# Recurrent attention in 64-token chunks with soft and dense MLP behind it: a round's products and transposes in another order

## The reference

```python
for t in range(S):                                   # the part that the change concerns
    cur = einsum('bhd,bhe->bhde', u * k[t], v[t])
    y[t] = einsum('bhd,bhde->bhe', r[t], state + cur)
    state = w[t][..., None] * state + einsum('bhd,bhe->bhde', k[t], v[t])
x = y as (3072, 384)
x = soft mixture of 8 experts (x, phi, w1, w2)       # softmax over tokens in, over slots out
out = relu(x @ w_in) ** 2 @ w_out                    # 3072 x 384
```

## Time and profile before

| | us |
|---|---|
| median of 3 runs | 546.54 (543.76 to 552.49) |
| the profiled execution | 547.0 |
| its span | 545.2 |
| attention rounds | from about 5 to 236 |
| mean granted clock of TensorE | 0.974 of full |

### The profile page before, as it was taken

One profiled execution on the slowest core, in us unless ns is written; L12 is line 12 of the kernel. 1 busy time (PEld: TensorE's weight loads), 2 busy tenths in 40 slices (PEclk: granted clock), 3 DMA queues, 4 the chain that ended last, 5 costly groups with the idle time before them and its releaser, 6 DMA issues.

```text
span 545.2 us, 18788 instructions
## 1 busy us (share of the span) xinstructions
PE 483.3 (89%) x7850; PEld 423.2 (78%) x7850; DVE 334.7 (61%) x583; ACT 332.6 (61%) x689; POOL 13.7 (3%) x21
## 2 busy tenths in 40 slices
PE   5868979798979798778798789999999999999996
PEld 3657768677867676777334289999999999999996
DVE  8687878786878788644441276555555555555552
ACT  4777686867777778353213276656565656565653
POOL 9000000000000000000000000000000000000000
PEclk9998999998999999789899979999999999999999
DMA  8775484846362624862999430101010101010101
GB/s 168 131 166 118 95 199 79 203 84 112 63 111 57 110 47 121 274 190 60 315 400 373 173 115 1 45 1 44 1 44 2 43 0 44 0 44 0 44 1 43
DMA packets 129388, 56.24 MB, mean 103 GB/s; under 512 B 103328, under 2 KB 128928, under 8 KB 128928
## 3 DMA queue, kind: packets, MB, share of 16 engines
q1 hardware_dynamic: 126112, 54.53, 38.1%
q10 hardware_dynamic: 3200, 0.59, 0.6%
HBM read 50.38 MB, written 4.72 MB: 101 GB/s over the span
## 4 chain that ended last, share of the span: by engine, by line
PE 74%; ACT 13%; issue 7%; DVE 3%; SPq 1%; ACTq 1%; DMA 0%; DVEq 0%
PE bank L730 12%; PE bank L732 12%; PE bank L731 12%; PE lbank L474 5%; ACT wide L825 5%; PE ybank L508 5%; PE bank L720 4%; PE ybank L524 4%; PE tbank L425 4%; PE lbank L491 3%; PE bank L669 2%; PE bank L646 2%; PE tbank L438 2%; ACT wl L766 2%; PE ybank L455 1%
## 5 line engine op out<-in xcount | busy, mean ns | idle before, releaser
L730 PE MATMUL bank<-wo_high,h_high 128*128 128x384 f32 x384 | 129.4, 337 | 1.6 <-DVE h_low L1228 1.4
L731 PE MATMUL bank<-wo_low,h_high 128*128 128x384 f32 x384 | 128.9, 336 | 0.0
L732 PE MATMUL bank<-wo_high,h_low 128*128 128x384 f32 x384 | 128.9, 336 | 0.0
L974 ACT ACTIVATE h_relu<-bank 128x384 f32<-128x384 f32 x128 | 62.9, 491 | 74.2 <-PE bank L720 73.7
L1226 DVE CAST h_high<-h_sq 128x384 fp32r<-128x384 f32 x128 | 46.0, 359 | 96.4 <-PE bank L732 87.7
L1062 DVE TENSOR_TENSOR rk<-rk,wl 112x768 f32<-112x768 f32 x80 | 76.2, 952 | 37.2 <-PE lbank L474 24.6
L730 PEld LDWEIGHTS bank<-wo_high,h_high 128*128 128x128 f32 x384 | 72.6, 189 | 3.0 <-issue 2.5
L1228 DVE TENSOR_TENSOR h_low<-h_sq,h_high 128x384 fp32r<-128x384 f32 x128 | 71.5, 558 | 4.4
L731 PEld LDWEIGHTS bank<-wo_low,h_high 128*128 128x128 f32 x384 | 72.5, 189 | 0.0
L732 PEld LDWEIGHTS bank<-wo_high,h_low 128*128 128x128 f32 x384 | 72.5, 189 | 0.0
L978 ACT ACTIVATE h_sq<-h_relu 128x384 f32<-128x384 f32 x128 | 67.4, 527 | 4.1
(11 more groups left out here) (123 smaller groups left out, 517.5 us busy)
## 6 DMA issues: line engine op xcount, KB each, us to landing
w_sb<-in_moe_w_dram SPq DMA_DIRECT2D x32, 384.0 KB, 5.3
w_hi<-in_moe_w_dram SPq DMA_DIRECT2D x16, 384.0 KB, 9.0
v_tok<-in_v_dram SPq DMA_DIRECT2D x32, 144.0 KB, 3.0
w_lo<-in_moe_w_dram SPq DMA_DIRECT2D x1, 4608.0 KB, 16.4
out_dram<-o_sb SPq DMA_DIRECT2D x8, 576.0 KB, 3.0
nat<-in_r_dram SPq DMA_DIRECT2D x62, 72.0 KB, 2.5
nat<-in_k_dram SPq DMA_DIRECT2D x62, 72.0 KB, 2.7
nat<-in_w_dram SPq DMA_DIRECT2D x60, 72.0 KB, 2.5
```

Source lines behind the costliest of these rows:

```text
L730: nc.tensor.matmul(acc, hi, wo_high[:, fb, :], start=(fb == 0), stop=False)
L731: nc.tensor.matmul(acc, hi, wo_low[:, fb, :], start=False, stop=False)
L732: last = nc.tensor.matmul(acc, lo, wo_high[:, fb, :], start=False, stop=(fb == NF - 1))
L974: nc.scalar.activation(h_relu[fb % 2][:], h_bank[fb % 2][:, 0:GT * P], ACT.Relu).then_inc(relu_done, 1)
```

## The change

The program text of PE, ACT and DVE is put in another order; no operation is added, removed or resized.

- PE: the near product of pair 0 moves from behind level 3 of pair 0 up to before level 2 of pair 1, its far product from behind level 3 of pair 1 to behind level 3 of pair 0, the near product of pair 1 from behind level 4 of pair 1 to before level 4 of pair 0, its far product from behind level 5 of pair 0 to behind level 4 of pair 1. The units slip down: unit 3 behind level 2 of pair 1, 5 behind level 3 of pair 0, 6 behind level 3 of pair 1, 7 behind level 4 of pair 0, 8 behind level 4 of pair 1, 9 and 10 behind level 5 of pair 0, and 11 behind level 5 of pair 1, the last thing of a round.
- ACT: its copies follow in the same order. Unit 11's copies now stand behind both pairs' level-5 copies, between those of pair 1 and the widening of pair 1.
- DVE: update 0 of pair 1 moves from the end of a round to the beginning of the next, behind merge 0 of pair 0.

```diff
@@ tensor, in the loop over rd
                 level(rd, 0, 2)
-                next_inputs(rd, 2, 2)
+                next_inputs(rd, 2, 1)
+                if late:
+                    y_near(rd - 1, 0)
                 level(rd, 1, 2)
-                next_inputs(rd, 4, 2)
+                next_inputs(rd, 3, 2)
                 level(rd, 0, 3)
                 if late:
-                    y_near(rd - 1, 0)
+                    y_far(rd - 1, 0)
+                next_inputs(rd, 5, 1)
+                level(rd, 1, 3)
                 next_inputs(rd, 6, 1)
-                level(rd, 1, 3)
                 if late:
-                    y_far(rd - 1, 0)
+                    y_near(rd - 1, 1)
+                level(rd, 0, 4)
                 next_inputs(rd, 7, 1)
-                level(rd, 0, 4)
-                next_inputs(rd, 8, 2)
                 level(rd, 1, 4)
                 if late:
-                    y_near(rd - 1, 1)
-                next_inputs(rd, 10, 1)
+                    y_far(rd - 1, 1)
+                next_inputs(rd, 8, 1)
                 level(rd, 0, 5)
-                if late:
-                    y_far(rd - 1, 1)
+                next_inputs(rd, 9, 2)
+                level(rd, 1, 5)
                 next_inputs(rd, 11, 1)
-                level(rd, 1, 5)
@@ scalar, the end of the loop over rd
-                top_level_out(rd, 0)
                 if late:
                     y_to_x(rd - 1, 1)
-                if ahead:
-                    inputs_out(rd + 1, 11, 1)
+                next_out(8, 1)
+                top_level_out(rd, 0)
+                next_out(9, 2)
                 if ahead:
                     widen(rd + 1, 0, 1)
                 top_level_out(rd, 1)
+                next_out(11, 1)
                 if ahead:
                     widen(rd + 1, 1, 1)
@@ vector
             for rd in range(ROUNDS):
-                for s in range(2):
-                    merge(rd, s, 0)
+                merge(rd, 0, 0)
+                if rd > 0:
+                    update(rd, 1, 0)
+                merge(rd, 1, 0)
...
                 for s in range(2):
                     update(rd, s, 5)
-                    if rd < ROUNDS - 1:
+                    if s == 0 and rd < ROUNDS - 1:
                         update(rd + 1, s, 0)
```

More of the change, by code:

```diff
@@ L863, in _, with next_out @@
                 late = rd > 0
+                def next_out(first, count):
+                    if ahead:
+                        inputs_out(rd + 1, first, count)
                 if late:
                     k_out(rd - 1, 0)
-                if late:
                     k_out(rd - 1, 1)
-                if late:
                     kv_out(rd - 1, 0)
-                if ahead:
-                    inputs_out(rd + 1, 0, 1)
+                next_out(0, 1)
                 widen(rd, 0, 2)
@@ L874, in _ @@
                     kv_out(rd - 1, 1)
-                if ahead:
-                    inputs_out(rd + 1, 1, 1)
+                next_out(1, 1)
                 widen(rd, 1, 2)
-                if ahead:
-                    inputs_out(rd + 1, 2, 2)
+                next_out(2, 1)
                 widen(rd, 0, 3)
-                if ahead:
-                    inputs_out(rd + 1, 4, 2)
+                next_out(3, 2)
                 widen(rd, 1, 3)
-                if ahead:
-                    inputs_out(rd + 1, 6, 1)
                 if late:
                     y_to_x(rd - 1, 0)
-                if ahead:
-                    inputs_out(rd + 1, 7, 1)
+                next_out(5, 2)
                 for s in range(2):
                     spread_w(rd, s)
[L892 to L895, removed]
-                top_level_out(rd, 0)
+                next_out(7, 1)
                 if late:
                     y_to_x(rd - 1, 1)
-                if ahead:
-                    inputs_out(rd + 1, 11, 1)
+                next_out(8, 1)
+                top_level_out(rd, 0)
+                next_out(9, 2)
                 if ahead:
```

## The result

| | before | after |
|---|---|---|
| median, us | 546.56 | 566.03 (564.51 to 566.93) |
| ratio | | 1.0353 (95% interval 1.0311 to 1.0394) |
| span of the profiled execution | 545.2 | 563.9 |
| mean granted clock | 0.974 | 0.940 |

A forecast was written before the change was run, and what follows sets the result against it. It took each attention round's end, a chain of small steps on three engines, as the bound, not PE work. Terms 8.5 + 0 - 0.6 = +7.9 on 547.0 gave 554.9, stated as 555.0 us; range 546 to 563.

The forecast's parts named there:

- The tail as a chain: Level-4 merge of pair 1 to next level 1 of pair 0: 8.45 us each, +8.5 over seven rounds' ends.
- The middle: Level 1 to level 4 of pair 0: +1.06 work against 1.07 waits, about 14 us unchanged; term 0, bounds ±0.5 a round.
- clock as before: Case of longer round ends at unchanged granted clock: 554.9 us by the sum, 551 to 559, chance 0.48.
- The clock: Rival, left out of the sum: clock falls at every round's end, +3 to +8.5 us, middle 560.6 us; chance 0.28.
- The last round: No units there; the near product covers a 0.96 us wait between levels 2: -0.6 us, ends -2.3 and +0.5.
- The issue pauses fall into idle time: TensorE pauses (0.95 and 1.38) that lengthened old round ends fall into idle time in new ones; already within the +8.5.
- gains win: Rival: rounds' ends are not the bound, removed waits are won, about 1.4 x 6 = 8 us: 539 us; chance 0.08.

The follow-up runs named there:

- the run with the pauses filled: Changed kernel with 14 and 7 identity transposes, read by nobody, added in the two TensorE pauses of each round's end: 552.70 us, 1.0141 of the kernel before.
- with the next one filled: Changed kernel with only the second pause of each round's end filled, by 7 identity transposes ahead of pair 1's k transposes: 555.60 us, 1.0165 of the kernel before.
- unit 11 alone: Kernel before with only unit 11 put behind level 5 of pair 1, its copies and update as in the change: 564.49 us, 1.0342.
- unit 11 back: Changed kernel with only unit 11, its copies and update put back to their old places: 552.57 us, 1.0127 of the kernel before.

## Why the prediction was wrong

- **The tail as a chain: right.** The sum was 8.45; with the clock held up it is 8.40 to 8.46 in seven tails, and in round 3 of the changed kernel each step up to the widening of pair 1 came within 0.02 us. What TensorE does inside it was read less well: it was busy 5.09 of the 7.48 us of the old tail, not "some 3 to 4".
- **The middle: nearly right at full clock.** I took 14.0, from one round, and had +1.06 of work against 1.07 of waits. The six rounds of before have 14.38 on the mean; with the clock held up it is 13.76, so the term was -0.6 a round, just past my bound of -0.5, and not 0.
- **The sum for "clock as before": near, with some luck.** 554.9 forecast, 552.70 measured where the pauses are filled. The profiled execution of that run, 550.66, has a span 3.7 longer than before and not 7.9, mostly for the middle term.
- **The clock: the step that failed.** "In the sum I leave it out and make a case of it", on the ground that five of seven tails of before had kept full clock. Counted behind level 5 of pair 1, those five tails had 1.4 to 1.9 us of pauses and the two at the low clock 1.7 and 2.1; I had computed 4.2 for the new ones, which is beyond all seven, and counted the old tails as evidence for them all the same. The runs show in its place a low stretch of 7 us at each of the seven ends, at 2.0 us a round. The rule of the Trainium skill that stood beside it ("TensorE: Matmul & The Clock Gate", HAM oscillation — how this bites in real kernels) was the one to go by: the clock fell at all seven ends. The case held 0.28 of the chance and should have been the likeliest.
- **Its price was too small as well.** I priced 0.6 to 1.7 a tail, level 1 and the k transposes at double duration, in five rounds. Measured are 2.0 a round, and in all seven, of which 1.47 lie in the middle of the next round: the low stretch lasts 7 us, not 3.5, since the second pause prolongs it, and behind level 1 TensorE works back to back, with nothing that could take it up. I had written myself that TensorE has no slack left in the middle, and still put the whole price into the tail. With 2.0 for seven rounds on the 554.9 the case gives 569, close to 566.
- **The last round:** -0.6 said. From level 1 of round 7 to the first transpose of x it is 27.5 instead of 26.15, +1.3. The near product does cover the wait for the widened copy. But levels 1 of both pairs and the first k times v run in the low stretch of the tail before, for 4.27 us instead of the 2.58 that they take in the run with the pauses filled, and two issue pauses of 1.93 and 2.64 stand where there was one of 2.30. In that run the stretch is 24.9, 1.2 less than before: the sign of the term was right there, and in the changed kernel the low clock and the pauses turn it round.
- **"The issue pauses fall into idle time": right,** 7.4 us of them instead of 14.3, and it was in the sum. Where one of 1.31 to 1.80 still stands ahead of the first wait of a tail, in rounds 3 to 5, that wait is 0.37 to 1.60 instead of 2.5, and the tail is no longer than the others.
- **The rival "gains win"** was priced at "about 1.4" a round; its own terms, 0.53 + 0.34 + 0.2 + 0.8, make 1.87, or 11 us instead of 8. Nothing hung on it.

## What to carry to other kernels

When a change adds idle time to TensorE, add the pauses of one place up and compare the sum with those that did and did not bring the low clock in the trace; if it is larger than all of them, the clock belongs into the sum, and with it the work that is queued behind, not only the step that follows. Below that the sum does not decide: of the old tails, one with 1.7 us of pauses went to the low clock and one with 1.9 did not. A unit that is moved last in a round is on the chain if its copy, its update and the next widening all have to come after it: the last place is free for the engine that issues it and dear for the ones that follow. And where an engine also has pauses that the profile cannot explain, count its instructions from the start of the program to each of them, in more than one version: if the counts agree, the pauses belong to the place and not to the work, and a wait that is removed can give back less than its length.

## What was not expected of the hardware

- 147 transposes that compute nothing made the kernel 13.3 us faster (566.03 to 552.70), by keeping the clock at 2.4 GHz.
- The low stretch at the first pause, with the next one filled, was 3.5 us long in five of six rounds, with both pauses open 7 us in all.
- TensorE's "issue" pauses add up to very different times in different orders of the same work: 2.7 us with unit 11 alone, 7.4 in the changed kernel, 14.3 before, 16.8 with unit 11 back. Yet they stand on one grid, a place every 125 or so recorded matmuls, in every version. What makes them was not tried.
